# Sketch matrix on ScalarE's DMA queue, four fillers, sketches ahead of attention pieces, query features in two halves

## The reference, cut to what matters

```python
def phi(x):                                  # S1, S2: 8 x 32 sketches
    a = einsum('rd,bhsd->bhsr', S1, x)
    b = einsum('rd,bhsd->bhsr', S2, x)
    return outer(a, b) over r                # 64 features
kv  = einsum('bhsf,bhsd->bhfd', phi(k), v);  z = sum(phi(k), axis=2)
att = einsum(phi(q), kv) / (einsum(phi(q), z) + 1e-6)       # -> x: (4, 1088, 128)
mixed = real(fft(fft(x, axis=1), axis=2));   u = x + mixed
x2 = u + relu(layernorm(u) @ w_ch1) @ w_ch2                 # 128 -> 512 -> 128
h  = relu(x2 @ w_in)                                        # 128 -> 1024
out = (h * sigmoid(conv3(h))) @ w_out                       # 1024 -> 128
```

## Time and profile before

| | |
|---|---|
| time, median of 3 runs | 265.8 us (265.61 to 266.71) |
| time of the profiled execution | 265.86 us |
| its span in the trace | 264.1 us |
| PE, weight loads, DVE, ACT busy | 250.1, 210.8, 219.2, 185.9 us |
| first stretch, to the last batch's key-value copies | 0 to 64.8 us |

### The profile page before, as it was taken

One profiled execution on the slowest core, in us unless ns is written; L12 is line 12 of the kernel. 1 busy time (PEld: TensorE's weight loads), 2 busy tenths in 40 slices (PEclk: granted clock), 3 DMA queues, 4 the chain that ended last, 5 costly groups with the idle time before them and its releaser, 6 DMA issues.

```text
span 264.1 us, 4307 instructions
## 1 busy us (share of the span) xinstructions
PE 250.1 (95%) x1524; PEld 210.8 (80%) x1524; DVE 219.2 (83%) x388; ACT 185.9 (70%) x357; POOL 27.0 (10%) x90
## 2 busy tenths in 40 slices
PE   8999999999999999998679999998999999999985
PEld 6989999989989989977567777776778677777753
DVE  0747978997998779795779989988799999998992
ACT  2351436333487454667989998999899989978872
POOL 0000000001513333238200000000000000000000
PEclk9999999999999999999999999999999999999999
DMA  6959730300000000000000000002000002002002
GB/s 191 388 206 350 282 95 0 93 4 0 2 0 2 1 1 2 0 2 2 0 0 0 2 0 0 1 2 84 0 0 2 0 0 84 5 0 84 0 0 84
DMA packets 4341, 13.04 MB, mean 49 GB/s; under 512 B 736, under 2 KB 1504, under 8 KB 4320
## 3 DMA queue, kind: packets, MB, share of 16 engines
q1 hardware_dynamic: 4320, 12.77, 13.2%
HBM read 10.54 MB, written 2.23 MB: 48 GB/s over the span
## 4 chain that ended last, share of the span: by engine, by line
PE 75%; ACT 13%; DVE 6%; issue 4%; ACTq 0%; DVEq 0%
PE ps L584 19%; PE ps L505 8%; PE ps L507 8%; PE ps L506 8%; PE ps L498 6%; PE ps L422 6%; PE ps L434 5%; ACT arena L773 4%; PE ps L463 4%; PE ps L545 3%; PE ps L447 3%; ACT arena L781 3%; ACT arena L786 2%; PE ps L590 2%; PE ps L484 2%
## 5 line engine op out<-in xcount | busy, mean ns | idle before, releaser
L584 PE MATMUL ps<-arena,wout 128*128 128x364 f32 (+1 forms) x192 | 62.8, 468 | 0.7 <-DVE arena L1005 0.7
L584 PEld LDWEIGHTS ps<-arena,wout 128*128 128x128 f32 x192 | 35.9, 189 | 20.8 <-issue 2.8
L993 DVE SCALAR_TENSOR_TENSOR arena<-arena,taps 128x1088 f32<-128x1088 f32 x32 | 43.2, 1349 | 4.5 <-ACT arena L781 4.5
L998 DVE SCALAR_TENSOR_TENSOR arena<-arena,taps 128x1088 f32<-128x1088 f32 x32 | 43.2, 1350 | 0.1
L773 ACT ACTIVATE arena<-ps 128x364 f32<-128x364 f32 x96 | 40.0, 479 | 3.8 <-PE ps L507 3.4
L1005 DVE TENSOR_TENSOR arena<-arena 128x1088 f32<-128x1088 f32 (+2 forms) x36 | 41.4, 1161 | 1.4 <-ACT arena L786 1.2
L505 PE MATMUL ps<-x2hi,wlo 128*128 128x364 f32 x96 | 38.8, 404 | 3.6 <-ACT arena L773 3.2
L781 ACT ACTIVATE arena<-arena,taps 128x1088 f32<-128x1088 f32 x32 | 38.7, 1209 | 0.6
L786 ACT ACTIVATE arena<-arena 128x1088 f32<-128x1088 f32 x32 | 35.5, 1111 | 1.9 <-DVE arena L998 1.9
L506 PE MATMUL ps<-x2lo,whi 128*128 128x364 f32 x96 | 31.5, 329 | 0.0
L507 PE MATMUL ps<-x2hi,whi 128*128 128x364 f32 x96 | 31.5, 328 | 0.0
(11 more groups left out here) (81 smaller groups left out, 420.0 us busy)
## 6 DMA issues: line engine op xcount, KB each, us to landing
arena<-v_d SPq DMA_DIRECT2D x4, 594.0 KB, 3.7
arena<-qT_d SPq DMA_DIRECT2D x3, 545.0 KB, 7.2
arena<-kT_d SPq DMA_DIRECT2D x3, 544.5 KB, 6.3
out_d<-arena SPq DMA_DIRECT2D x3, 544.0 KB, 2.7
cos_t<-cos_d SPq DMA_DIRECT2D x1, 926.5 KB, 5.6
sin_t<-sin_d SPq DMA_DIRECT2D x1, 926.5 KB, 7.4
arena<-qT_d SPq DMA_DIRECT2D x2, 272.5 KB, 4.6
wraw<-w_d SPq DMA_DIRECT2D x2, 256.0 KB, 5.4
```

The source lines that it names most:

```text
L584: pe.matmul(ps[:, OUT_BANK + t, 0:z - a], wout[:, c, :], gate[:, i % GATES, a:z], start=(c == 0), stop=(c == C2 - 1)).then_inc(wout_done, 1)
L993: dve.scalar_tensor_tensor(out=gate[:, i % GATES, 1:S + 1], in0=h2[:, i % HIDDENS, 0:S], scalar=taps[:, i % C2, 0:1], in1=gate[:, i % GATE ...
L998: dve.scalar_tensor_tensor(out=gate[:, i % GATES, 1:S + 1], in0=h2[:, i % HIDDENS, 2:S + 2], scalar=taps[:, i % C2, 2:3], in1=gate[:, i % ...
```

## The change

Five edits:

1. The load of `sketch` moves from the head of SP's list to the head of ACT's.
2. `WARM_UP` is 4 instead of 5.
3. For b = 0 and 1, `sketches(b + 2)` piece n is issued ahead of `attend(b, n)`, not behind it.
4. `query_features` is issued in two halves of 5 tiles. The first group of transposes waits for the first half, and the third group, the first to read the second half, for both.
5. `normalise(b)` is cut in two: the first piece is normalised by itself between the two halves of the query features (in the last batch between `mixed_rows(1)` and `moments(1)`), and the other three pieces follow.

```diff
--- before.py
+++ after.py
@@ -70,7 +70,7 @@
 NC1 = (D1 // 128) * NR
 NI = B * (D2 // 128)
 EPS = 1e-6
-WARM_UP = 5
+WARM_UP = 4
 LOW_UNTIL = NC1 // 2 + 2
 
 
@@ -100,6 +100,7 @@
 ET_PIECES = [(0, 4), (4, 5)]
 SP_PIECES = [(0, 3), (3, 5)]
 TR_PIECES = 5
+Q_PARTS = ((0, 5), (5, 10))
 
 
 def build(nc, kT_d, qT_d, v_d, s_d, ident_d, chan_d, cos_d, sin_d, w1_d, w2_d, win_d, wout_d, cw_d, out_d):
@@ -330,7 +331,6 @@
                     sp.wait_ge(kv_done, b)
                 sp.dma_start(v1[:], v_d[:, b]).then_inc(ld_v, 16)
 
-            sp.dma_start(sketch[:], s_d).then_inc(ld_sketch, 16)
             load_sketched(0)
             load_sketched(1)
             load_values(0)
@@ -439,7 +439,9 @@
 
             def feature_transposes(b, n):
                 if n == 0:
-                    pe.wait_ge(qphi_ready, b + 1)
+                    pe.wait_ge(qphi_ready, 2 * b + 1)
+                if 2 * n + 1 >= Q_PARTS[0][1] > 2 * n - 1:
+                    pe.wait_ge(qphi_ready, 2 * b + 2)
                 bank = bank_of["features", b, n]
                 claim(bank, (qphiT_ready, TR_PIECES * b + n + 1))
                 for y in range(4):
@@ -603,9 +605,9 @@
                 if b >= 1:
                     fold_transposes(b - 1)
                 for n in range(len(AT_PIECES)):
-                    attend(b, n)
                     if b + 2 < B:
                         sketches(b + 2, KQ_PIECES[n:n + 1])
+                    attend(b, n)
                 if b >= 1:
                     channel_spectra(b - 1)
             for n in range(TR_PIECES):
@@ -650,7 +652,7 @@
                     kq_turn[0] += 1
                     act.wait_ge(sk_done, n + 1)
                     if b >= 1 and t0 == 0:
-                        act.wait_ge(kphi_ready if side == 0 else qphi_ready, b)
+                        act.wait_ge(*((kphi_ready, b) if side == 0 else (qphi_ready, 2 * b)))
                     ab, rows = (ab_k, TK) if side == 0 else (ab_q, TQ)
                     act.activation(ab[:, t0:t1].rearrange("p t h r -> p (t h r)"),
                                    ps[0:rows, bank_kq(n), 0:(t1 - t0) * H * AB], ACT.Copy).then_inc(ab_ready, 1)
@@ -736,6 +738,7 @@
                     normed_high(r + 1)
 
 
+            act.dma_start(sketch[:], s_d).then_inc(ld_sketch, 16)
             act.wait_ge(ones_ready, 1)
             act.activation(spare[:], warm[:, 0:1], ACT.Sigmoid)
             sketch_copies(0)
@@ -832,11 +835,12 @@
                     dve.wait_ge(kv_done, b - 1)
                 features(b, ab_k, kphi[:, b % 2], NK, kphi_ready)
 
-            def query_features(b):
+            def query_features(b, part):
+                t0, t1 = Q_PARTS[part]
                 dve.wait_ge(ab_ready, 4 * b + 4)
                 if b >= 1:
                     dve.wait_ge(tr_done, TR_PIECES * b)
-                features(b, ab_q, qphi, NQ, qphi_ready)
+                features(b, ab_q[:, t0:t1], qphi[:, t0:t1], t1 - t0, qphi_ready)
 
             def block_diagonal(b):
                 dve.wait_ge(kv_done, b + 1)
@@ -848,27 +852,41 @@
                 dve.tensor_copy(kvz[0:F, :, 0:V1], src[0:F, :, 0:V1])
                 dve.tensor_copy(kvz[F:2 * F, :, V1:2 * V1], src[F:2 * F, :, V1:2 * V1]).then_inc(kvz_ready, 1)
 
-            def normalise(b):
-
-                pieces = len(AT_PIECES)
-                banks = [bank_of["attention", b, n] for n in range(pieces)]
-                for n in range(pieces + 1):
-                    if n < pieces:
-                        t0, t1 = AT_PIECES[n]
-                        src = ps[0:TQ, banks[n], 0:(t1 - t0) * H * V1].rearrange("p (t c) -> p t c", c=V1)
-                        r = rden[:, t0:t1, :].rearrange("p t h -> p (t h)")
-                        dve.wait_ge(att_done, pieces * b + n + 1)
-                        dve.tensor_scalar(r, src[:, :, D], EPS, None, ALU.add).then_inc(den_ready, 1)
-                    if n >= 1:
-                        u0, u1 = AT_PIECES[n - 1]
-                        src = ps[0:TQ, banks[n - 1], 0:(u1 - u0) * H * V1].rearrange("p (t c) -> p t c", c=V1)
-                        q = rden[:, u0:u1, :].rearrange("p t h -> p (t h)")
-                        dve.wait_ge(rden_ready, pieces * b + n)
-                        dve.tensor_tensor(x_nat[:, b, u0:u1, :].rearrange("p t (h d) -> p (t h) d", d=D), src[:, :, 0:D],
-                                          q.unsqueeze(2).broadcast_to([TQ, (u1 - u0) * H, D]), ALU.mult).then_inc(x_ready, 1)
-                    if n < pieces:
-                        dve.wait_ge(den_ready, pieces * b + n + 1)
-                        dve.reciprocal(r, r).then_inc(rden_ready, 1)
+            def divided(b, n):
+
+                t0, t1 = AT_PIECES[n]
+                bank = bank_of["attention", b, n]
+                src = ps[0:TQ, bank, 0:(t1 - t0) * H * V1].rearrange("p (t c) -> p t c", c=V1)
+                return (src[:, :, 0:D], src[:, :, D], rden[:, t0:t1, :].rearrange("p t h -> p (t h)"),
+                        x_nat[:, b, t0:t1, :].rearrange("p t (h d) -> p (t h) d", d=D))
+
+            def denominators(b, n):
+                _, den, r, _ = divided(b, n)
+                dve.wait_ge(att_done, len(AT_PIECES) * b + n + 1)
+                dve.tensor_scalar(r, den, EPS, None, ALU.add).then_inc(den_ready, 1)
+
+            def reciprocals(b, n):
+                _, _, r, _ = divided(b, n)
+                dve.wait_ge(den_ready, len(AT_PIECES) * b + n + 1)
+                dve.reciprocal(r, r).then_inc(rden_ready, 1)
+
+            def quotients(b, n):
+                num, _, r, x = divided(b, n)
+                dve.wait_ge(rden_ready, len(AT_PIECES) * b + n + 1)
+                dve.tensor_tensor(x, num, r.unsqueeze(2).broadcast_to([TQ, r.shape[1], D]), ALU.mult).then_inc(x_ready, 1)
+
+            def normalise_first(b):
+                denominators(b, 0)
+                reciprocals(b, 0)
+                quotients(b, 0)
+
+            def normalise_rest(b):
+                for n in range(1, len(AT_PIECES)):
+                    denominators(b, n)
+                    if n >= 2:
+                        quotients(b, n - 1)
+                    reciprocals(b, n)
+                quotients(b, len(AT_PIECES) - 1)
 
             def mirror_fold(b):
                 here, there = x_nat[:, b, 0:NJ, :], x_nat[:, b, NJ:NQ, :]
@@ -961,15 +979,18 @@
 
             dve.memset(warm, 1.0).then_inc(ones_ready, 1)
             key_features(0)
-            query_features(0)
+            query_features(0, 0)
+            query_features(0, 1)
             for b in range(B - 1):
                 key_features(b + 1)
                 if b == 2:
                     weight_low(0, 0, D1)
                     weight_low(1, D1, 2 * D1)
                 block_diagonal(b)
-                query_features(b + 1)
-                normalise(b)
+                query_features(b + 1, 0)
+                normalise_first(b)
+                query_features(b + 1, 1)
+                normalise_rest(b)
                 mirror_fold(b)
                 if b >= 1:
                     partner_fold(b - 1)
@@ -978,8 +999,9 @@
             moments(0)
             block_diagonal(B - 1)
             mixed_rows(1)
+            normalise_first(B - 1)
             moments(1)
-            normalise(B - 1)
+            normalise_rest(B - 1)
             normed_low(0)
             mirror_fold(B - 1)
             partner_fold(B - 2)
```

## The result

The changed kernel takes 264.34 us (median of 5 executions from 263.94 up) against 266.71 for the kernel before on the same chip: a ratio of 0.9925, with a 95% interval from 0.9901 to 0.9949 (the comparison's estimate; the two medians alone would give 0.991). That is faster by 0.5 to 1.0%. The profiled execution took 264.67 us, with a span of 262.9 us, 1.2 us less than the 264.1 before.

A forecast was written before the change was run, and what follows sets the result against it. PE was taken as the bound, busy 250.1 of 264.1 us, so only its idle places could be won. Start -0.40, edit 3 -0.48, batch 2 +0.05, last batch -0.10 sum to -0.93: 265.86 becomes 264.9 us, range 264.0 to 266.1.

The forecast's parts named there:

- the likeliest case: Whole kernel: the terms hold as summed, -0.93 us to 264.9, own range 264.6 to 265.4; chance 0.55.
- signs of being wrong: First transposes gain over 0.6 us or nothing; batch 2's next transposes move under 0.4 or over 1.3; drift behind 74 us.
- signs of the mechanism: Sketches at 4.7 us, slow until 5.4; no idle at batch 0's seam; batch 2 wait of 0.8 us at `L486`, none at `L465`.
- start, to the first transposes: Edits 1 and 2: one filler fewer gains PE 0.47 us, 0.15 if keys land no earlier; -0.40 taken.
- edit 3, to batch 2's copies: Sketches cover PE's idle at the seams of batches 0 (-0.65 us) and 1 (-0.20), less a price of 0.37: -0.48.
- edits 4 and 5, batch 2: The 0.78 us wait ahead of attention piece 3 only moves to the spectra, as 0.84 us: +0.05.
- last batch: DVE's 0.24 us idle for piece 3 goes, two overlapped pairs lose some 0.07 each: -0.10 us.
- the rest: From 74 us on both kernels have one list on every engine, so what was gained stays: 0.
- The landings: At the start, SP issues every other load 0.43 us earlier; batch 1's keys would land at 8.92 instead of 9.35 us.
- its price: Attention piece 3 ends 0.96 us later: 0.07 us lost at batch 0's spectra, DVE 0.30 late at batch 2's copies; +0.37.
- The case in which the gains add up: DVE not late at batch 2, half of the 0.78 us won, start at -0.50: -1.9 us, 264.0; chance 0.22.
- The rival on the other side: Clock rises later at the start, each microsecond costing 0.5 us until the sketches end; 8.5 gives 266.5 us; chance 0.10.

The follow-up runs named there:

- five fillers and the pieces first: Changed kernel with WARM_UP = 5; in batch 2 the other three pieces are normalised ahead of the query features' second half, and two folds swapped: 264.20 us, ratio 0.9926.
- the one at 263.7: Changed kernel, keeping four fillers, with batch 2's other three pieces normalised ahead of the second half of the query features: 263.70 us, ratio 0.9903; a sixth execution took 295.69.

## Why the prediction was right, and where it was off

The forecast was 264.9 us in a range of 264.0 to 266.1, and 264.34 lies in it. As a change it was worse: I had 0.35% and a chance of 0.23 for a gain over 0.5%, and 0.75% came. That the time still lies in the range is in part luck, and it lies below the 264.6 to 265.4 that the likeliest case had for itself.

The forecast also named its own signs of being wrong, and by its letter all three came: the first transposes gained 0.71 us (over 0.6), batch 2's next transposes moved by 1.36 (over 1.3), and the kernels drifted apart by 0.26 us behind 74 us. The signs of the mechanism came as told: sketches at 4.75 with slow loads until 5.5, no idle time at batch 0's seam, DVE at batch 2's copies out of its own list, 1.0 us of idle at `L486` for `L876` and no wait for the bank within `L465`. So the path was right and its sizes were too small, the start's above all.

The sum was made against the profiled execution, so its terms are best read there:

| term | predicted | measured |
|---|---|---|
| start, to the first transposes | -0.40 (-0.50 to -0.15) | -0.71 |
| edit 3, to batch 2's copies | -0.48 | -0.74 |
| edits 4 and 5, batch 2 | +0.05 | +0.09 |
| last batch | -0.10 | -0.11 |
| the rest | 0 | +0.26 |
| sum | -0.93 | -1.21 |

- **The start** was undersized, beyond its own bounds. PE's gain from the filler itself was sized rightly: the sketch loads ran at half pace from 4.3 to 5.5, and DVE's features began 0.39 us earlier (0.47 forecast). What was missed is that PE in the kernel before wasn't quite busy to the transposes: it starts them 0.1 us behind the end of its last sketch load, where in the changed kernel it starts them 0.12 ahead. That is 0.2 us lost to the features, as the rows of edits 1 and 2 show too, and edit 4 removes it. I wrote that PE needs only the first half at once and gave it no number. Some 0.1 more came from the keys: I read that PE had up to 0.15 us of slack on them, but between 9.2 and 9.4 us its loads are busy for only 0.13 of 0.20 us, so it already waited for them. Together, 0.39, 0.2 and 0.1 make the 0.71.
- **The landings** moved by 1.0 us in the changed kernel, not by the 0.43 of one issue. They scatter from run to run, though: 9.35, 9.2 and 8.9 us in the three profiles with the sketch on SP's queue, and in the ten with it on ACT's 7.7 to 8.9 in nine and 9.9 in one, with means of 9.1 and 8.3. SP issues the load 0.48 us earlier; with this scatter it isn't shown that the move of the sketch gives more than that.
- **Edit 3's gain** was undersized and its price oversized. The stretch from the first transposes to batch 1's spectra fell by 1.01 us (28.32 to 27.31) where I had 0.85. The price was smaller: 0.07 at the copies (0.27 of idle against 0.20), 0.14 at the spectra (1.30 for loads that take 1.16) and 0.06 at the transposes behind them: 0.27 against 0.37. DVE's lateness at the copies, 0.30 in the sum, is the 0.07. The mechanism, DVE late at batch 2's copies because attention piece 3 comes later, was as told.
- **Batch 2** came out as worked: first product in time, 1.01 us of idle at the spectra (0.84 forecast), next transposes 6.52 us behind the copies (6.49 forecast; 6.43 before). That the second half of the features is the cause is shown by the kernel that moves it. The case in which the gains add up came near by its number, but half of it only: DVE was hardly late, and of the 0.78 us nothing was won.
- **The last batch** was right to 0.01 us.
- **The clock** fell once behind 130 us, 0.26 us that the sum didn't have. From the last fold to the end, the kernels without the fall took 190.02 us (before) and 189.93 (edits 1 and 2), those with it 190.08 to 190.35. So the 0.26 fits the fall, but the fall alone doesn't cost a fixed amount, and why it comes in one execution and not in another of nearly the same work is open.
- **The late clock.** The rival on the other side was right as a mechanism and wrong in size and chance. By its rate of half a microsecond per microsecond a rise at 75 us would cost (75 - 5.45) x 0.5 = 35 us, and 32 came; what I hadn't thought of is that the clock can stay down far beyond the sketches. It gives no slower median, but one execution in four of the four-filler kernels takes 32 us more. As a mean over executions edit 2 is a loss: 10/37 x 32 = 8.6 us against a gain that the comparison of four and five fillers puts at 0.8 us (265.20 to 264.39) and 0.5 (264.20 to 263.70), both across two chips. On one chip, ahead of edits 3 to 5, it was 0.1 us: 265.61 with edit 1, 265.49 with both.
- **What remains.** The ratio of 0.9925 is 2.0 us on 266.71, more than the 1.2 us between the two profiles. The kernel before spans 265.3 to 267.1 us, and its profile, at 265.86, is at the lower end of the five executions it was compared with. When the changed kernel was run again, beside 14 executions of the kernel before with a median of 265.88, the ratio was 0.9933. The mean granted clocks on record add something: of 68 executions of the kernel before, the 30 with 1.000, like its profile, lie around 265.6 us, and the 38 with 0.994, as a fall like the one behind 130 us gives, around 266.5, while all executions of the changed kernel near 264.3 have 0.993 or 0.994. Beside those with a fall it gains 2.2 us. The fall itself costs at most 0.33 us in the profiles, and in the kernel with five fillers and the pieces first the executions with 1.000 are the longer ones (264.4 against 264.0), so the clock's part in this isn't shown.

## What to carry to other kernels

- An idle time that is due to an order on another engine moves with that order. Ask, for the engine that is waited for, what its list does next: here half of the features, put between two products, only carried PE's 0.8 us wait from one bank to the next, and moving it behind them won 0.9 us.
- Fillers at the start aren't only cover for a load. Judge their number by all executions and not by a median, and by what runs behind them; the best version to keep here is the one with five fillers and the pieces first, at 264.2 us, not the one at 263.7.
- When two things end at about the same time in a trace, the one that ends last by 0.2 us is the next term of the sum.

## What the runs showed of the hardware

The time at which TensorE's clock rises differs from execution to execution of one kernel and of nearly equal ones: at 5.45 us before, and at 5.5, 6.2, 6.5, 4.2 and 4.1 in others, read from where fillers and sketch loads turn from some 330 ns to 176 to 190. With five fillers the first transposes come later by half of the delay (13.41, 13.77 and 13.93 us for rises at 5.45, 6.2 and 6.5). By this rate, rises from 4.1 to 6.5 us would spread the times by 1.2 us, as an estimate from these profiles; the executions of the kernel before spread by 1.8 (265.26 to 267.06), and their rises aren't on record.

A PE that is busy all the time doesn't bring the clock up by itself. In a stretch of short matmuls (64, 66 and 109 columns, with a load ahead of each) and loads busy for 19.25 us of 20, it stayed at 1.2 GHz from the start to 75 us in two profiles, and from 11.5 us for more than 80 in a third, in which it had already been at 2.4 GHz and two gaps of 0.56 and 0.36 us came first. How often this happens with three, four, five and six fillers I have seen only as counts; what sets it off isn't settled.
